# Both expert stages as plain fp32 products in two column halves

## What is computed

```python
def _attn_ref(q, k, v, tau):
    scores = scale * np.matmul(q, k.transpose(0, 1, 3, 2))
    thresh = np.max(scores, axis=-1, keepdims=True) - tau
    scores = np.where(scores >= thresh, scores, -1000000000.0)
    ...
    return np.matmul(attn, v).astype(np.float32)

def _moe_ref(x, w_gate, w1, w2):          # N, D, E, F = (2304, 512, 8, 1024)
    expert_idx = np.argmax(x @ w_gate, axis=1)
    ...
    for e in range(E):
        xe = x[expert_idx == e]
        h = np.maximum(xe @ w1[e], 0.0)
        ye = h @ w2[e]
        out[mask] = gate_w[mask, None] * ye

def _moe2_ref(x, domain_probs, w1, w2):   # N, D, E, F = (2304, 512, 4, 1024)
    p = domain_probs / (domain_probs.sum(-1, keepdims=True) + 1e-09)
    for e in range(E):
        h = np.maximum(x @ w1[e], 0.0)
        out += p[:, e:e + 1] * (h @ w2[e])
```

## Time and profile before

| | us |
|---|---|
| median of three runs | 1391.9 (1391.07 to 1392.91) |
| the profiled execution, its own time | 1392.69 |
| its span, first to last instruction | 1391.0 |
| attention, routing, and the start of the first expert stage | 0 to 341.06 |
| first expert stage on PE | 341.06 to 638.91 |
| second expert stage on PE | 638.91 to 1387.49 |

### The profile page before, as it was taken

One profiled execution on the slowest core, in us unless ns is written; L12 is line 12 of the kernel. 1 busy time (PEld: TensorE's weight loads), 2 busy tenths in 40 slices (PEclk: granted clock), 3 DMA queues, 4 the chain that ended last, 5 costly groups with the idle time before them and its releaser, 6 DMA issues.

```text
span 1391.0 us, 27885 instructions
## 1 busy us (share of the span) xinstructions
PE 1370.9 (99%) x10213; PEld 1201.4 (86%) x10213; DVE 989.9 (71%) x1492; ACT 672.7 (48%) x1163; POOL 182.1 (13%) x329
## 2 busy tenths in 40 slices
PE   8999999998999999999999999999999999999999
PEld 6777777777888888899898989889898989989897
DVE  7888888865877777798756657884756687584762
ACT  5777777763666666665323324442322444142320
POOL 3222222212122222251000000200000020000000
PEclk9999999999999999999999999999999999999999
DMA  4322323214988889942120312311120322111111
GB/s 93 69 66 60 68 61 70 54 27 124 332 289 280 283 293 303 345 160 107 62 96 28 119 61 77 136 61 61 61 103 26 128 74 93 61 62 62 59 61 46
DMA packets 170165, 160.67 MB, mean 116 GB/s; under 512 B 89808, under 2 KB 122672, under 8 KB 170096
## 3 DMA queue, kind: packets, MB, share of 16 engines
q1 hardware_dynamic: 163072, 140.65, 32.1%
q0 software_dynamic: 5824, 18.83, 3.8%
q10 hardware_dynamic: 1200, 0.26, 0.1%
HBM read 143.58 MB, written 16.12 MB: 115 GB/s over the span
## 4 chain that ended last, share of the span: by engine, by line
PE 94%; DVE 2%; ACT 1%; issue 1%; DMA 1%; POOL 0%; SPq 0%; ACTq 0%; DVEq 0%; POOLq 0%
PE front L1224 6%; PE front L1223 6%; PE front L1222 6%; PE back L818 6%; PE back L1152 6%; PE back L1154 6%; PE back L1153 6%; PE front L843 4%; PE front L1092 3%; PE front L1094 3%; PE front L1093 3%; PE back L1223 3%; PE back L1224 3%; PE back L1222 3%; PE front L856 2%; PE front L1154 2%
## 5 line engine op out<-in xcount | busy, mean ns | idle before, releaser
L1152 PE MATMUL back<-x2h,w1h 128*128 128x384 f32 x480 | 160.8, 335 | 0.2 <-DVE two L1940 0.2
L1154 PE MATMUL back<-x2h,w1l 128*128 128x384 f32 x480 | 160.5, 334 | 0.0
L1153 PE MATMUL back<-x2l,w1h 128*128 128x384 f32 x480 | 160.4, 334 | 0.0
L1224 PE MATMUL front<-dn_h,h2l 128*128 128x512 f32 x384 | 149.8, 390 | 0.0
L1223 PE MATMUL front<-dn_l,h2h 128*128 128x512 f32 x384 | 149.7, 390 | 0.0
L1222 PE MATMUL front<-dn_h,h2h 128*128 128x512 f32 x384 | 149.6, 389 | 0.0
L1498 ACT COPY one<-front 128x384 f32<-128x384 f32 x48 | 22.6, 472 | 206.7 <-PE front L1154 197.8
L772 POOL DMA_INDIRECT out<-rows,out_i x15 | 20.0, 1334 | 698.2 <-DVE rows L1932 696.4
L818 PEld LDWEIGHTS back<-vv,pt 128*64 128x64 f32 x2840 | 89.3, 137 | 13.1 <-issue 13.1
L818 PE MATMUL back<-vv,pt 128*64 128x65 f32 x2840 | 100.2, 224 | 0.0
L1816 DVE TENSOR_TENSOR w1l<-w1r,w1h 128x1024 fp32r<-128x1024 f32 x84 | 97.6, 1218 | 0.0
(11 more groups left out here) (296 smaller groups left out, 3625.2 us busy)
## 6 DMA issues: line engine op xcount, KB each, us to landing
early<-in_moe_w SPq DMA_DIRECT2D x64, 512.0 KB
ring<-in_moe_w SPq DMA_DIRECT2D x64, 512.0 KB
w1r<-in_moe_w SPq DMA_DIRECT2D x48, 512.0 KB, 3.7
dn_r<-in_moe_w SPq DMA_DIRECT2D x48, 512.0 KB, 5.8
tokens_x<-x_nat SPq DMA_DIRECT2D x16, 288.0 KB, 4.5
raw<-in_q SPq DMA_DIRECT2D x32, 128.0 KB, 2.6
vv<-in_v SPq DMA_DIRECT2D x32, 128.0 KB, 2.2
raw<-in_k SPq DMA_DIRECT2D x30, 128.0 KB, 2.7
```

The source lines that it names most:

```text
L1152: pe.matmul(to[:, 0:CH], w1h[:, w, kk, fs], x2h[:, x, kk, :], start=start and kk == 0, stop=False, skip_group_check=not start)
L1153: pe.matmul(to[:, 0:CH], w1h[:, w, kk, fs], x2l[:, x, kk, :], start=False, stop=False, skip_group_check=not start)
L1154: last = pe.matmul(to[:, 0:CH], w1l[:, w, kk, fs], x2h[:, x, kk, :], start=False, stop=kk == 1, skip_group_check=not start)
L1224: last = pe.matmul(to, h2l[:, f, ts], w2_block(dn_h, f), start=False, stop=n == KF - 1)
```

## The change

Every block of both expert stages becomes one plain fp32 matmul, issued as two with 64 stationary columns each, which write partitions 0 to 63 and 64 to 127 of the same bank. All low parts, the instructions that made them, their buffers and semaphores go. What was a copy to fp32r on ACT is a copy to fp32. The slots of one tile use `up` like the others, with 128 moving columns, and `turn_h` and its two ACT steps go. PE waits on ACT's copies (`s_wh`, `s_x2`, `s_hh`, `s_ah`, `s_bh`, `s_w2h`). DVE gets a small `keep_tab` in place of `x_lo`. SP's reloads wait for ACT's copy; in the second stage it fetches the next expert's four up pieces together, in the order A21, A22, A11, A12. Buffers that are gone are replaced by spaces, so that the others keep their place.

```diff
+            def full(to, w, x, start, stop, skip=False):
+
+                for c in range(2):
+                    cs = slice(c * HALF, (c + 1) * HALF)
+                    last = pe.matmul(to[cs, :], w[:, cs], x, start=start, stop=stop, skip_group_check=skip)
+                return last
...
                     for kk in range(KD):
-                        pe.matmul(hb(f, n), w1_block(up_h, kk, f), xch[:, kk, 0:n], start=kk == 0, stop=False)
-                        pe.matmul(hb(f, n), w1_block(up_h, kk, f), xcl[:, kk, 0:n], start=False, stop=False)
-                        last = pe.matmul(hb(f, n), w1_block(up_l, kk, f), xch[:, kk, 0:n], start=False, stop=kk == KD - 1)
+                        last = full(hb(f, n), w1_block(up_h, kk, f), xch[:, kk, 0:n], kk == 0, kk == KD - 1)
...
-                        pe.matmul(acc_bank[t], hth[:, f, ts], w2_block(dn_h, f), start=f == 0, stop=False)
-                        pe.matmul(acc_bank[t], hth[:, f, ts], w2_block(dn_l, f), start=False, stop=False)
-                        last = pe.matmul(acc_bank[t], htl[:, f, ts], w2_block(dn_h, f), start=False, stop=f == KF - 1)
+                        last = full(acc_bank[t], hth[:, f, t * P:(t + 1) * P], w2_block(dn_h, f), f == 0, f == KF - 1)
...
-                if single(m, b):
-                    up_single(m, j)
-                else:
-                    up(j, j, n * P)
+                up(j, n * P, tiles_to(m, b) + n)
...
                 for kk in range(2):
-                    pe.matmul(to[:, 0:CH], w1h[:, w, kk, fs], x2h[:, x, kk, :], start=start and kk == 0, stop=False, skip_group_check=not start)
-                    pe.matmul(to[:, 0:CH], w1h[:, w, kk, fs], x2l[:, x, kk, :], start=False, stop=False, skip_group_check=not start)
-                    last = pe.matmul(to[:, 0:CH], w1l[:, w, kk, fs], x2h[:, x, kk, :], start=False, stop=kk == 1, skip_group_check=not start)
+                    last = full(to[:, 0:CH], w1h[:, w, kk, fs], x2h[:, x, kk, :], start and kk == 0, kk == 1, not start)
...
-                        pe.matmul(to, h2h[:, f, ts], w2_block(dn_h, f), start=n == 0, stop=False)
-                        pe.matmul(to, h2h[:, f, ts], w2_block(dn_l, f), start=False, stop=False)
-                        last = pe.matmul(to, h2l[:, f, ts], w2_block(dn_h, f), start=False, stop=n == KF - 1)
+                        last = full(to, h2h[:, f, ts], w2_block(dn_h, f), n == 0, n == KF - 1)
```

More of the change, by code:

```diff
@@ L275, in build @@
         sb = pool_of(ctx)
[L276 to L278 removed]
+        w1r, w1h = (sb(n, [P, 7, 2, FF // 2]) for n in ("w1r", "w1h"))
         front = ctx.enter_context(nc.psum_tensor("front", [P, 4, 512], F32))
@@ L1095, in down @@
                         if f == KF - 1:
                             last.then_inc(done, 1)
-                    if pair and f in (1, 3, 5):
-                        last.then_inc(s_half, 1)
                     if closing and f == 1:
                         last_rows()
-            def up_single(m, g):
-                pe.wait_ge(s_xl, g + 1)
-                for a in range(2):
-                    pe.wait_ge(s_wl, NP * g + 2 * a + 2)
-                    for kk in range(KD):
-                        if a == 1 and kk == 2:
-                            turn_h(m, 0)
-                        pe.matmul(S[0][:, a, :], xch[:, kk, 0:P], w1_half(up_h, kk, a), start=kk == 0, stop=False)
-                        pe.matmul(S[0][:, a, :], xch[:, kk, 0:P], w1_half(up_l, kk, a), start=False, stop=False)
-                        last = pe.matmul(S[0][:, a, :], xcl[:, kk, 0:P], w1_half(up_h, kk, a), start=False, stop=kk == KD - 1)
-                    last.then_inc(s_u, KF // 2)
@@ L1115, in turn_h @@
-            def turn_h(m, a):
-                pe.wait_ge(s_hn, 2 * m + a + 1)
-                for i in range(4):
-                    last = pe.transpose(S[1][:, a, i * P:(i + 1) * P], hn(a)[:, i, :], ident[:])
-                last.then_inc(s_ht, 1)
             def slot(m, b):
                 n, j = tiles_of(m, b), 2 * m + b
-                if single(m, b):
-                    up_single(m, j)
-                else:
-                    up(j, j, n * P)
+                up(j, n * P, tiles_to(m, b) + n)
@@ L1131, in slot @@
                     turn_x(*after(m, b))
-                if single(m, b):
-                    turn_h(m, 1)
                 if not (isinstance(m, int) and m == 0 and b == 0):
                     pe.wait_ge(s_y, tiles_to(m, b))
-                down(j, j, n, s_dn, pair=b == 0 and not final(m, b), closing=final(m, b))
+                down(j, n, s_dn, closing=final(m, b))
             turn_x(0, 0)
             idle_turns(12, TP)
+            pe.wait_ge(s_cnt, 1)
             slot(0, 0)
@@ L1912, in _ @@
             slot(LAST, 1)
-            w_rest(0, 3)
-            w_rest(0, 4)
             x_mixes(0)
-            for i in range(6):
-                x_rest(0, i)
             def add_up(p, e, half):
```

236 lines of the change are left out of this document (55 added, 181 removed).

## The result

The changed kernel takes **1642.0 us** (median of three runs, 1641.84 to 1642.35) where the kernel before takes 1391.9: a ratio of 1.180, 95% interval 1.177 to 1.182. The forecast was 1644.6 in 1630 to 1688, slower. Its profiled execution took 1642.0 with a span of 1640.3.

A forecast was written before the change was run, and what follows sets the result against it. PE, busy 99% of the span, was the bound, through distances between its matmul starts: 340.6 before the expert stages + 363.1 + 936.5 + 3.5 after = 1643.7 span, with 0.9 over the span 1644.6 us; range 1630 to 1688.

The forecast's parts named there:

- The price of a pair: Expert matmuls on PE: two column-half records together take 0.429 us at 512 columns, 0.3225 at 384, 0.216 at 256, 0.1095 at 128.
- The stages: PE's time in the two expert stages: first 363.1 us (297.85 before), second 936.5 us (748.58 before).
- The changes: PE switching between full array and column halves in the expert stages: 0.3 us for both ways, 17 places in the first.
- The 1.8 us kept in the second stage: Second expert stage: measured 748.58 us before against 746.8 summed from rows; the difference was kept, giving 936.5.
- the 7 us in the first stage: First expert stage before: measured 297.85 us against 290.9 summed; 1.67 a wait for `htl`, the rest put on weight-bound 256-column distances.
- The start: PE's first expert matmul: at 340.6 us instead of 341.06, no longer held up 0.42 by DVE's second `xcl`.
- Excess on plain records: Expert matmuls: plain records also carry fp32r's 14 ns over the ticks, 43 us more, 1688; chance 0.07.
- Stalls in single slots: First expert stage: ACT's relus behind 1.05 us copies hold PE in seven one-tile slots, 17 us, 1662; chance 0.06.
- the margin named for them: Each one-tile slot of the first expert stage: PE takes 15.1 us, ACT 12.7, leaving 2.4 us.
- Exposed loads: Expert matmuls: each pair's weight loads wait for matmuls in flight, 0.06 us each, 235 us in all, 1880; chance 0.03.
- Halves one after the other: Expert matmuls: the two column halves do not run side by side, doubling the 1273.5 us product part, 2918; chance 0.02.
- one pass for each record: Expert matmuls: a wide column half needs one tick per column, product part 637 us, total 1008, not slower; chance 0.02.

The follow-up runs named there:

- the run that was meant to bring this delay back: The changed kernel with two DVE subtractions put back at the start of the first expert stage, their result unused; 1650.33 us.

## Why the prediction was right

**The price of a pair** carried it, and held: the distances between starts, added up over all records of a shape, are 667.0 us for 512 columns (forecast 171.8 + 494.8 = 666.6), 433.7 for 384 (433.4), 125.3 for 256 (124.4) and 49.6 for 128 (49.1); the measured sums contain the late starts beside each change of halves, 0.05 to 0.1 us each. Few rows of the kernel before were enough, since plain fp32 in full clock and in halves was already there.

**The stages**: 362.74 against 363.1, and 934.28 against 936.5. The changes were priced at 0.3 and cost it (0.10 to the first transpose, 0.06 to the second, 0.09 to the next pair, 0.05 to the pair after it), 21 of them. The 0.4 in each stage are the third decimal of the pairs' price (0.8584 for a block of 512 columns where I took 0.859). The 1.8 us kept in the second stage belong to fp32r: over the whole stage before, its records stand at 0.1740 and 0.2274 us where five and eighteen of them gave 0.1735 and 0.227, and nothing of that is there with plain fp32 (934.28 against a sum of 934.7). Rightly, nothing was carried over of the 7 us in the first stage: `htl` is waited for no more, and the fp32r records of 256 columns, 0.113 in the earlier trace rows, stand at 0.118 in most of the stage: 864 of them take 103.7 us, not 97.6. The 0.113 were read in its first 7 us. That the loads of weights hold them there, as I wrote, no run shows.

**The start**: the forecast took away the 0.42 us for `xcl` and left the gather alone. It was 0.8 us too late, by the gather that DVE's low part had held up, as the rows read; the run that was meant to bring this delay back did not. That is the one step with a missing mechanism. **The tail** was 3.5 as said.

**The rivals.** Excess on plain records (1688): no, 429 ns for pairs and for full-width records alike. Stalls in single slots (1662): no, and the margin named for them was the wrong measure; the runs with doubled copies show that ACT could carry 8 us more in each slot. The point from which it decides would be the due time of a copy, not the sum over a slot. The stops that do come there on some chips are worth 8 us and are none of ACT's. Exposed loads (1880): no, spoke rightly against the rule. The section of the Trainium skill that the prediction names ("TensorE: Matmul & The Clock Gate", "Part 3: Packing small matmuls") has more than the prediction took from it: a load is also pulled ahead when it targets the background weight buffer. The loads on all rows beside matmuls without a pause agree with that; which way they go no run here shows. Halves one after the other (2918) and one pass for each record (1008): no.

The sum errs by 2.6 us in all: 0.8 of the start, 0.4 and 2.2 of the stages, less 0.8 that lies outside the span (1.7 us in this profiled execution where I took 0.9). That the last cancels the first is luck.

## What to carry to other kernels

When PE has no idle time, ask only how many passes a block takes and what distance each pass keeps; taking hundreds of microseconds from DVE gains nothing until PE's passes shrink below DVE's own sum. Column halves on a product that fills the array are two halves of the same price, and each change between them and the full array, there and back, costs 0.3 us. If a product is made of high and low parts, try bf16 for the parts first: the same three passes cost 5% less here than with fp32r (the whole kernel 3.9%), though two bf16 parts hold 16 significant bits of an operand, which has to be enough.

To see whether an engine's work is covered, compare each step's end with the time at which its reader wants it; a sum over a stretch overstates the danger.

## What was not expected of the hardware

- fp32r records keep 12 to 15 ns over their ticks (0.1185 us at 256 columns, 0.1737 at 384, 0.228 at 512, without DVE's low parts), bf16 and plain fp32 records some 2.5 (at the same three widths bf16 0.1093, 0.1625, 0.216, plain fp32 0.216, 0.3225, 0.429). Why fp32r has more was not found. fp32r in column halves was not tried.
- At 128 columns an fp32r record and a plain full-width one both keep 0.111 to 0.112 us, though the fp32r one has half the ticks.
- POOL's issue of a gather or scatter, 0.96 to 1.0 us alone (the first gather 1.23 in every kernel), took up to 1.98 when it began during a subtraction of DVE with two operands in SBUF.
- A stream of two records in 0.109 us was stopped twice per 128 records on two chips, 1.0 us in most single slots, and not on two others and in the session of the result, one of the programs being the same.
